# Gathers issued one macro earlier, four banks for a chain of transposes, and filler transposes on an idle TensorE

## The reference

```
attention:  16 heads (2 x 8), 768 tokens, head size 64. Each q and k gets a 6-bit bucket from the signs
            of q @ proj; scores count only where the buckets are equal; softmax; times v.
            The result is x: 1536 tokens x 512.
layer 0:    xn @ en.T / tau -> softmax over 8 experts -> best expert and its probability g
            x2[token] = g * (relu(x @ w1[e]) @ w2[e])              w1: 512 x 1024, w2: 1024 x 512
layer 1:    logits = x2 @ w_gate + log1p(exp(x2 @ w_noise)) * noise -> best two of 8 experts, softmax of the two
            out[token] = sum over the two of weight * (relu(x2 @ w1[e]) @ w2[e])
```

## Time and profile before

| | us |
|---|---|
| runs shown, median | 944.32 (938.66, 944.32, 944.51) |
| the profiled execution, its own time | 936.66 |
| its span, first to last instruction | 934.9 |
| mean granted clock of TensorE, share of full speed | 0.945 |
| attention | 0 to 281.7 |
| first routing | to 299.8 |
| layer 0's experts | to 506.3 on TensorE |
| x2 back, transposes and logits | to 535.9 |
| rest of the second routing | to 559.7 |
| layer 1's experts | to the end |

### The profile page before, as it was taken

One profiled execution on the slowest core, in us unless ns is written; L12 is line 12 of the kernel. 1 busy time (PEld: TensorE's weight loads), 2 busy tenths in 40 slices (PEclk: granted clock), 3 DMA queues, 4 the chain that ended last, 5 costly groups with the idle time before them and its releaser, 6 DMA issues.

```text
span 934.9 us, 12557 instructions
## 1 busy us (share of the span) xinstructions
PE 814.9 (87%) x4560; PEld 650.9 (70%) x4560; DVE 521.0 (56%) x884; ACT 423.3 (45%) x689; POOL 249.4 (27%) x247
## 2 busy tenths in 40 slices
PE   4899999999990789999996617998989898989997
PEld 2566666666650679999985407787789787879795
DVE  4787877877747566666663385343255362436221
ACT  5667776777763444544442414242143241424110
POOL 2000000000001324444451007144264462536331
PEclk9899999999996799999999857998999999999999
DMA  5415212220002756666665306335173561345110
GB/s 176 167 69 190 73 59 87 103 81 4 21 1 76 275 187 226 228 224 227 223 222 192 105 0 197 111 93 191 36 259 112 192 237 68 112 170 161 56 47 34
DMA packets 50039, 123.62 MB, mean 132 GB/s; under 512 B 10337, under 2 KB 12385, under 8 KB 49712
## 3 DMA queue, kind: packets, MB, share of 16 engines
q1 hardware_dynamic: 35488, 87.21, 27.8%
q0 software_dynamic: 12032, 29.02, 8.9%
q10 hardware_dynamic: 2448, 6.46, 1.8%
HBM read 109.34 MB, written 17.92 MB: 136 GB/s over the span
## 4 chain that ended last, share of the span: by engine, by line
PE 67%; DVE 9%; DMA 7%; POOL 7%; issue 6%; ACT 2%; POOLq 1%; ACTq 0%; DVEq 0%; SPq 0%
PE ps L1224 25%; PE ps L1242 11%; PE ps L1051 8%; PE ps L1074 7%; PE ps L1060 6%; DMA xm<-x_tokens,idx_m 4%; PE ps L1268 2%; POOL ym L364 2%; PE ps L1196 2%; POOL gate_m L364 2%; PE ps L1041 2%; PE ps L1087 1%; DMA raw<-in_moe_w 1%; DVE row_low L719 1%; DMA xm<-x_tokens,ids 1%
## 5 line engine op out<-in xcount | busy, mean ns | idle before, releaser
L579 ACT ACTIVATE w_hi<-raw 128x1024 fp32r<-128x1024 f32 x124 | 129.2, 1055 | 94.1 <-PE ps L1224 74.9
L916 DVE TENSOR_TENSOR w_lo<-raw,w_hi 128x1024 fp32r<-128x1024 f32 x120 | 145.7, 1226 | 39.4 <-ACT w_hi L579 39.0
L1242 PE MATMUL ps<-xTm_hi,w_hi 128*128 128x256 f32 (+1 forms) x512 | 159.9, 312 | 2.9 <-ACT xTm_hi L567 2.9
L1242 PE MATMUL ps<-xTm_lo,w_hi 128*128 128x256 f32 (+1 forms) x512 | 159.5, 312 | 0.0
L1242 PE MATMUL ps<-xTm_hi,w_lo 128*128 128x256 f32 (+1 forms) x512 | 159.4, 311 | 0.0
L1224 PE MATMUL ps<-w_hi,hT_hi 128*128 128x512 f32 x320 | 131.2, 410 | 3.2 <-DVE hT_lo L926 3.2
L1224 PE MATMUL ps<-w_lo,hT_hi 128*128 128x512 f32 x320 | 127.7, 399 | 0.0
L1224 PE MATMUL ps<-w_hi,hT_lo 128*128 128x512 f32 x320 | 127.4, 398 | 0.0
L719 DVE TENSOR_REDUCE row_low<-ps 128x1 f32<-128x768 f32 x96 | 91.7, 955 | 45.3 <-PE ps L1051 44.7
L1051 PEld LDWEIGHTS ps<-K,Q 128*128 128x128 f32 (+1 forms) x384 | 67.6, 196 | 63.0 <-issue 34.9
L471 ACT ACTIVATE probs<-ps,exp_in 128x768 f32<-128x768 f32 x96 | 95.2, 991 | 22.1 <-DVE exp_in L723 21.4
(11 more groups left out here) (225 smaller groups left out, 1157.6 us busy)
## 6 DMA issues: line engine op xcount, KB each, us to landing
raw<-in_moe_w SPq DMA_DIRECT2D x128, 512.0 KB, 4.8
rows_K<-in_k SPq DMA_DIRECT2D x8, 768.0 KB, 4.3
rows_Q<-in_q SPq DMA_DIRECT2D x8, 768.0 KB, 5.8
v<-in_v SPq DMA_DIRECT2D x8, 384.0 KB, 3.5
out<-xr ACTq DMA_DIRECT2D x1, 3072.0 KB, 14.7
x_tokens<-x_sb ACTq DMA_DIRECT2D x2, 1536.0 KB, 5.1
x_sb<-x_tokens SPq DMA_DIRECT2D x12, 256.0 KB, 5.2
K<-row_bits_K SPq DMA_DIRECT2D x24, 24.0 KB
```

The costliest lines, as they stand in the source:

```text
L579: a.activation(w_hi[E % 2][:, c, :], raw[:, c % RING, :], ACT.Copy).then_inc(split_hi, 1)
L916: v_.tensor_tensor(w_lo[E % 2][:, c, :], raw[:, c % RING, :], w_hi[E % 2][:, c, :].bitcast(f32), ALU.subtract).then_inc(split_lo, 1)
L1242: last = te.matmul(ps[:, n % UP_BANKS, j * TW:(j + 1) * TW], w_[par][:, kk, f], x_[:, kk, 0:TW], start=(kk == 0 and m == 0), stop=(kk == K ...
```

## The change

Three things are changed.

1. GpSimd gathers the x of a macro one macro earlier. macro_x(1) stands right behind macro_x(0), and macro_x(e + 2) in macro e's loop of scatters, ahead of the last tile's. It reads its place in `ids` with `rest_before`, a load of a register. `idx_m` gets a fourth buffer, and the wait for the scatters that read one moves with it.
2. x2's transposes use four banks (t % 4) instead of two.
3. `keep_clock(n)` issues n transposes of the identity into bank 0, whose result nothing reads: 44 of them ahead of x2's transposes, 24 in each layer ahead of the first macro's x transposes (behind the wait for `routed`).

```
-        idx_m = [sb(f"idx_m{i}", [P, MTX], i32) for i in range(3)]
+        idx_m = [sb(f"idx_m{i}", [P, MTX], i32) for i in range(4)]
...
+        X2_BANKS = 4
...
                 def macro_x(e, r0):
                     if e:
                         wait(s["xm_ps"], MT * e)
-                        for h in range(MT if e > 3 else 0):
-                            wait(s[f"ym_out{h}"], 16 * (e - 2))
-                        g.tensor_copy(idx_m[e % 3][:, 0:MT], ids[:, bass.ds(r0 + MT * e, MT)]).then_inc(s["idx_m"], 1)
+                        for h in range(MT if e > 4 else 0):
+                            wait(s[f"ym_out{h}"], 16 * (e - 3))
+                        g.tensor_copy(idx_m[e % 4][:, 0:MT], ids[:, bass.ds(r0 + MT * e, MT)]).then_inc(s["idx_m"], 1)
...
                 macro_x(0, r0)
+                macro_x(1, rest_before(pool, L, 1))
...
                     r1 = rest_before(pool, L, e + 1)
-                    if e + 1 < NX:
-                        macro_x(e + 1, r1)
...
                     for h in range(MT):
                         wait(s["ym_ev"], MT * e + h + 1)
                         scatter(y_rows, column(e, h), ym[h][:], s[f"ym_out{h}"])
+                        if h == MT - 2 and e + 2 < NX:
+                            macro_x(e + 2, rest_before(pool, L, e + 2))
...
+            def keep_clock(n):
+                for _ in range(n):
+                    te.transpose(ps[:, 0, 0:P], ident[:], ident[:])
...
                 if L:
+                    keep_clock(44)
                     pe.wait_ge(gate_split, 2)
                     for t in range(NT):
                         pe.wait_ge(x2_in[t], 16)
-                        if t >= 2:
-                            pe.wait_ge(rx_ev, t - 1)
+                        if t >= X2_BANKS:
+                            pe.wait_ge(rx_ev, t - X2_BANKS + 1)
                         for kk in range(KD):
-                            last = te.transpose(ps[:, t % 2, kk * P:(kk + 1) * P], x_sb[:, t, kk * P:(kk + 1) * P], ident[:])
+                            last = te.transpose(ps[:, t % X2_BANKS, kk * P:(kk + 1) * P], x_sb[:, t, kk * P:(kk + 1) * P], ident[:])
...
+                keep_clock(24)
                 for h in range(MT):
                     x_macro(0, h)
```

More of the change, by code:

```diff
@@ L376, in column @@
                 def column(e, h):
-                    return (idx_m[e % 3] if e else ids)[:, h:h + 1]
+                    return (idx_m[e % 4] if e else ids)[:, h:h + 1]
                 def macro_x(e, r0):
@@ L629, in _ @@
                 a.activation(x2T_hi[t // LG % 2][:, :, t % LG * P:(t % LG + 1) * P],
-                             ps[:, t % 2, :].rearrange("p (k n) -> p k n", n=P), ACT.Copy).then_inc(rx_hi, 1)
+                             ps[:, t % X2_BANKS, :].rearrange("p (k n) -> p k n", n=P), ACT.Copy).then_inc(rx_hi, 1)
                 if t > LG and t % LG == 1:
@@ L824, in x2_low @@
                 w = slice(t % LG * P, (t % LG + 1) * P)
-                v_.tensor_tensor(x2T_lo[t // LG % 2][:, :, w], ps[:, t % 2, :].rearrange("p (k n) -> p k n", n=P),
+                v_.tensor_tensor(x2T_lo[t // LG % 2][:, :, w], ps[:, t % X2_BANKS, :].rearrange("p (k n) -> p k n", n=P),
                                  x2T_hi[t // LG % 2][:, :, w].bitcast(f32), ALU.subtract).then_inc(rx_ev, 1)
```

## The result

The changed kernel takes 910.39 us (median of 4 runs, 908.38 to 914.04), the kernel before, timed beside it, 943.47 us (938.66 to 944.51): a ratio of 0.9663, 95% interval 0.9616 to 0.9711. That is 33.1 us less. The prediction was 916, in a range of 909 to 927. The profiled execution took 911.48 us, with a span of 909.7 in place of 934.9; between the two profiles lie 25.2 us, where the prediction's sum was 26.4.

A forecast was written before the change was run, and what follows sets the result against it. The prediction took TensorE to bound the kernel, busy 814.9 of 934.9 us, with idle waits and low clock to win. Terms -23.2, -2.9 and -0.3 sum to -26.4; moved to the median that gave 916 us, range 909 to 927.

The forecast's parts named there:

- the prediction's sum: Whole kernel: the savings of the three changes added, -26.4 us, from the profiled 936.66 to 910.3 us.
- Part 1: Macro x gathers issued one macro earlier: all seven waits for x go, and the low clock behind them; -23.2 us.
- The clock behind them: TensorE behind the waits for x: products and transposes at lowered clock return to full speed; -5.9 us.
- The delay of the third scatter: GpSimd's queue: moved gathers start the third scatter 0.5 to 1.5 us late; cost zero, bound 0 to +1 us.
- Part 2: Second routing, x2's transposes: four banks and 44 fillers ahead save 2.9 us, bounds -4 and +2.
- the clock would stay up: x2's transposes: the 44 fillers end 2.7 us before x2 lands and the clock holds; -3.1 us, otherwise -2.6.
- what a full clock would give: x2's transposes at full clock: 3.2 us plus 1.3 of bank waits, less 1.4 for ScalarE and VectorE; -3.1 us.
- Part 3: 24 fillers before each layer's first x transposes: 0 in the first layer, -0.3 us overall, bounds -2.2 and +0.8.
- 1, the next wait takes over: Late y gathers or index copy behind the scatters lose half the moved gathers' gain; 927 us, chance 0.09.
- 2, it doesn't do what it says: Waits for x end as before, since something other than queue place holds the gather; 941 us, chance 0.03.
- 3, fillers keep the clock wherever they are: Fillers hold the clock up before x2's and each layer's first x transposes; 913 us, chance 0.07.
- 4, slower by y behind the scatter: Six second-layer macros: late y makes TensorE wait for its output bank once y lands after 742.4; chance 0.03.

The follow-up runs named there:

- dense_fill: Changed kernel with more filler transposes wherever TensorE waits, from layer 0's last product to the second layer's first; 906.64 us, ratio 0.9596.
- x_only: Changed kernel without filler transposes and with two banks for x2, so only the gathers are moved; 914.22 us, ratio 0.970.
- no_fill: Changed kernel without its 44 and 24 filler transposes: moved gathers and four banks only; 911.97 us, ratio 0.9654.
- after: Changed kernel with all three changes, first profile; median 910.39 us, ratio 0.9663 to the kernel before.
- after_again: Changed kernel, no edit, timed and profiled once more; 909.67 us, ratio 0.9620.
- delay8: Changed kernel with ten useless GpSimd fills ahead of the third scatter in each second-layer macro; 909.69 us, ratio 0.9655.
- delay16: Changed kernel with twenty useless GpSimd fills ahead of the third scatter in each second-layer macro; 917.98 us, ratio 0.9742.
- before_again: Kernel before the change, no edit, timed and profiled again; 942.30 us, ratio 0.9993.
- before: Kernel before the change, unedited, first profile, the one the prediction was read from; profiled execution 936.66 us.
- part2_only: Kernel before with four banks for x2's transposes and the 44 fillers, gathers not moved, no 24 fillers; 943.72 us, ratio 1.0002.
- fill24_only: Kernel before with only the 24 fillers ahead of each layer's first x transposes, two banks, gathers not moved; 943.02 us, ratio 0.999.

## Why the prediction was right

**Part 1: right in mechanism, size too small.** -23.2 us was predicted. Against the trace that it was read from, the second layer gives 365.5 less 341.7, -23.8, and every step is in the rows above: all seven waits gone, the clock up to the end, no new wait. That trace was a lucky one, though. Against the mean of four the layer gives -26.8, and the kernel with the gathers alone runs 28.9 us below the kernel before. Two terms were too small. The waits were 17.3 us in the one trace, and 19.4 on average over both layers. The clock behind them was 5.9 us in the sum; by the slow busy time it is 6.4 in that trace and 8.1 on average. Some of the rest is in the first layer, where the wait for x by idx_m was 0.23 us in the first profile, but 1.1, 1.9, 0.4 and 1.9 in the others with gathers one macro ahead, and none with them moved.

**The delay of the third scatter** was put at 0.5 to 1.5 us. The scatter starts 1.4 us after VectorE's output instead of 0.8, so it is 0.6 late. That this costs nothing is shown beyond its bound: 6.3 us more cost nothing either. The moved gathers took 1.00 to 1.07 us, as the rows said, where the gates that now start beside VectorE's splits take up to 2.06. The Trainium skill's "SBUF — State Buffer" ("Who interferes with whom"), by which a VectorE instruction with two SBUF inputs stands in the way of GpSimd's reads, fits both.

**Part 2: too large.** -2.9 predicted; by the table 22.19 less 21.14, -1.0 against the first trace. The 44 ran at full clock (4.97 us) and left 2.43 us, as worked out. Two steps failed. The first is that the clock would stay up. x2's third tile had not landed, so TensorE waited 1.23 us more for it, and the clock fell at 516.4 after all. It fell in each of the six profiles with these 44, for 3.4 us in two, 6.8 in two and 10.2 in two, and with it the stretch spreads from 21.14 to 24.16. I had priced that case at -2.6 against the first trace; the mean of the six is 22.3, against 23.2 for the five with two banks, less than either spreads. The second is what a full clock would give. Even with the clock up throughout, as in dense_fill, the stretch takes 20.65 us, 1.5 less than in the first trace instead of 3.1. Its chain goes through the arrival of the tiles (the fourth is transposed at 515.40, behind its landing) and then through ScalarE and VectorE to each group's logits. I had discounted 1.4 us for that and should have discounted 3.

**Part 3: right.** -0.3 predicted; from the sum to the first product -0.4 against the first trace, 0.5 in the mean of six profiles with the 24 (33.02, dense_fill left out) against six without (33.51). In the changed kernel's profile the second layer's 24 ran at the lower clock to their end (5.36 us, 0.22 each); the clock rose at 564.2, as they ended, and fell again at 567.6, 0.4 us before the first product. The Trainium skill's "TensorE: Matmul & The Clock Gate" ("HAM oscillation — how this bites in real kernels") has such a fall in the waits between bursts; by it the part gives nothing, and what little it gives is in the x transposes before the fall.

**From the sum to the median.** The sum was -26.4, the two profiles differ by 25.2, the medians by 33.1. I took 916 between 917.9 and 914, arguing that runs with worse luck gain more. That argument held and went further than I let it: the profiled execution was among the fastest of the kernel before, and the gain in the median is nearer to the gain over the mean of executions. The bounds that I named for the range add up to 911 to 926.5 around 916, not to 909 to 924, so at 910.4 the result is within the stated range by less than 2 us, and just outside what its terms give. Of the 33.1 the table's means account for 26.8 in the second layer, about 1 in x2's stretch and 0.5 in the start. x2's first transpose comes at 514.6 on average in the four profiles with the old gathers and nothing in the waits, and at 512.0 in x_only, no_fill, after and after_again: 2.6 us, of which 0.9 are the waits for x in the first layer. That leaves some 2 us that are not pinned down. The rest of the 2.6 may be chance: that time differs with the weight loads at the first layer's start (512.3 to 518.7 with the old gathers, 510.5 to 513.9 with the moved ones). Whether the moved gates have a part in it wasn't tried.

**The rivals.** 1, the next wait takes over: fell, by the lists of after and by delay8. 2, it doesn't do what it says: fell, x_only. 3, fillers keep the clock wherever they are: not these 68, but dense ones do, for 2.4 us. 4, slower by y behind the scatter: the kernel is far from it, and delay16 names another place than I did. The rest tile's y reaches its limit first, not a macro's, and TensorE stands in the next up pass, not for its output bank.

## What to carry to other kernels

A gather that is late by 3 us in an in-order queue may need no more than a place further up. Putting it ahead of work with slack gave in this layer what a whole macro of lead gave; look for what is queued ahead of it and how late that may be. Size a wait that ends with a DMA from several executions, since one trace gave 17.3 us of a mean of 19.4. Where the clock follows the waits the fastest execution hides part of the gain. Price the clock by the busy time in its low stretches, not by what fillers win, since fillers lengthen a wait that is shorter than they are. Fillers pay where they leave no rest behind them, and only by what TensorE itself would have done faster.

## What the runs showed of the hardware

A rest of about the same length lowers the clock in one execution and not in another. Rests of 3.25 us (before_again, at 739.08) and 3.39 (before, at 734.88) were spared, and so was one of 2.64; rests of 2.78 us (part2_only, at 782.77), 2.86 (at 836.23) and 3.32 (fill24_only, at 737.59) were not. When it fell, it came back in some cases after 3.4 us and in others after 6.8, though TensorE was busy for 4.7 of 6 us then. With these chances and the waits' own spread, runs of the same kernel differ by up to 15 us, and 44 or 24 transposes in the wrong stretch move nothing that a time can show.

Gathers and scatters on GpSimd are slower beside VectorE's weight splits. In the kernel before 81 of them overlap no split and take 1.07 us at most, 1.01 on average; the 97 that overlap one take 1.47 on average. In the changed kernel it is 1.02 (87 of them) against 1.53 (91).
